# Moving two SBUF buffers of a fused attention and feed-forward kernel by 64 bytes, and what lies behind them by 256

## What is computed

```python
k_p = k.reshape(B, H, 72, 8, D).mean(axis=3)          # v_p likewise
attn = softmax(q @ k_p.T / sqrt(D)) @ v_p
h = x @ w_in;  g = maximum(0.01 * h, h);  y = g @ w_out          # layer 1
h = y @ w_in2; g = h * clip(h + 3, 0, 6) / 6;  out = g @ w_out2  # layer 2
```

## Time and profile before

| | us |
|---|---|
| median of three runs | 1704.76 |
| lowest, highest | 1704.0, 1704.78 |
| the profiled execution | 1704.56 |
| its span, first to last instruction | 1702.8 |
| TensorE matmuls busy | 1675.4 (98%) |
| VectorE busy | 1007.7 (59%) |
| ScalarE busy | 627.9 (37%) |
| GpSimd busy | 395.3 (23%) |

### The profile page before, as it was taken

How to read it: one execution, slowest core, us unless ns; L and a number is a source line. 1 busy time by engine, 2 the same in 40 slices (tenths; PEclk the granted TensorE clock), 3 DMA queues, 4 the chain that set the end, 5 groups by cost and what they waited for, 6 DMA issues and landing times. The chain is left out here.

```text
span 1702.8 us, 32933 instructions
## 1 busy us (share of the span) xinstructions
PE 1675.4 (98%) x10460; PEld 1489.4 (87%) x10460; DVE 1007.7 (59%) x1807; ACT 627.9 (37%) x1329; POOL 395.3 (23%) x427
## 2 busy tenths in 40 slices
PE   7999999999999999999999999999999999999999
PEld 6777888888888888888999888988989898989898
DVE  6767777676676867765455555444545454444444
ACT  4544433333333433333323333333333333333333
POOL 6226551021120212112432112121111212121200
PEclk8999999999999999999999999999999999999999
DMA  6745778768686786858787757666756675757562
GB/s 197 244 154 195 260 253 247 234 202 278 197 260 222 227 261 204 273 179 280 234 271 245 251 174 227 175 222 176 223 180 222 174 226 174 227 173 227 173 202 75
DMA packets 215810, 366.83 MB, mean 215 GB/s; under 512 B 22464, under 2 KB 47040, under 8 KB 215744
## 3 DMA queue, kind: packets, MB, share of 16 engines
q1 hardware_dynamic: 215744, 366.04, 68.1%
HBM read 308.28 MB, written 57.67 MB: 215 GB/s over the span
## 5 line engine op out<-in xcount | busy, mean ns | idle before, releaser
L1431 PE MATMUL ps_h<-xs_hi,ring 128*128 128x256 f32 x3808 | 814.8, 283 | 10.6 <-ACT p L1056 4.9
L1431 PEld LDWEIGHTS ps_h<-xs_hi,ring 128*128 128x128 f32 x3808 | 642.8, 189 | 56.4 <-issue 15.9
L1431 PE MATMUL ps_h<-xs_lo,ring 128*128 128x256 f32 x1904 | 534.3, 281 | 0.0
L1431 PEld LDWEIGHTS ps_h<-xs_lo,ring 128*128 128x128 f32 x1904 | 358.1, 188 | 25.7
L939 ACT ACTIVATE g_hi<-gate 128x512 fp32r<-128x512 f32 x288 | 181.9, 632 | 397.7 <-DVE gate L1137 212.7
L1384 PE MATMUL ps_y<-g_hi,wout_hi 128*128 128x512 f32 x576 | 225.7, 392 | 0.4 <-DVE y_stage L1192 0.4
L1386 PE MATMUL ps_y<-g_hi,wout_lo 128*128 128x512 f32 x576 | 225.4, 391 | 0.0
L1385 PE MATMUL ps_y<-g_lo,wout_hi 128*128 128x512 f32 x576 | 225.2, 391 | 0.0
L1196 DVE TENSOR_TENSOR u<-ps_h,p 128x256 f32<-128x256 f32 x272 | 114.3, 420 | 186.8 <-PE ps_h L1431 152.1
L1385 PE MATMUL ps_y<-wout_lo,g_hi 128*128 128x512 f32 x576 | 224.2, 389 | 0.0
L1386 PE MATMUL ps_y<-wout_hi,g_lo 128*128 128x512 f32 x576 | 224.2, 389 | 0.0
(11 more groups left out here) (115 smaller groups left out, 1994.2 us busy)
## 6 DMA issues: line engine op xcount, KB each, us to landing
ring<-w_in_split SPq DMA_DIRECT2D x920, 256.0 KB, 2.8
w_in_split<-ring SPq DMA_DIRECT2D x56, 256.0 KB, 3.5
w_in_split<-stage SPq DMA_DIRECT2D x56, 256.0 KB, 3.6
k_raw<-in_kT SPq DMA_DIRECT2D x32, 288.0 KB, 3.8
q_raw<-in_qT SPq DMA_DIRECT2D x32, 288.0 KB, 5.3
v_raw<-in_v SPq DMA_DIRECT2D x32, 288.0 KB
x0T<-x_stage SPq DMA_DIRECT2D x32, 288.0 KB, 3.8
x1T<-y_stage SPq DMA_DIRECT2D x36, 256.0 KB, 5.0
```

Source lines behind the costliest of these rows:

```text
L1431: mm = pe.matmul(banks[BANK_OF[r]], a, b[:, r, c, :], start=r in OPENS and c == 0 and n == 0, stop=c == 1 and n == 2, skip_group_check=True)
```

## The change

Sixteen float32 per partition (64 bytes) are allocated ahead of `g_hi`, and 48 (192 bytes) ahead of `x_stage`. Nothing reads or writes them. No instruction is added, removed or reordered.

```diff
         pre = sb("pre", [P, 2, N])
+
+        sb("pad_g", [P, 16])
         g_hi = sb("g_hi", [P, G_SLOTS, N], F32R)
         g_lo = sb("g_lo", [P, G_SLOTS, N], F32R)
+        sb("pad_x", [P, 48])
         x_stage = sb("x_stage", [P, DC, N])
```

## The result

The changed kernel takes 1712.61 us in the median of six runs (1712.09 to 1718.89), the kernel before 1704.77 us (six runs, 1704.0 to 1706.82). The ratio is 1.0049, with a 95% interval of 1.0038 to 1.006: slower by 0.5%, inside the forecast's range and against its likeliest case. The profiled execution has a span of 1711.5 us, 8.7 more than before, at a mean granted clock of 0.995 of full speed (0.996 before), so the clock is not what changed.

What follows compares the result with a forecast made beforehand. TensorE's matmuls, busy 98% of the span, were taken as the bound, so time is their number times the distance between starts. All terms were 0 against 1704.56 us; forecast 1704.7 us, likeliest case 1703 to 1707, whole range 1688 to 1720.

Steps and rivals of the forecast that it cites:

- likeliest case: Whole kernel: no effect on TensorE's pace, 1703 to 1707 us, chance 0.50.
- What writes g on ScalarE and VectorE: g_hi's copy and g_lo's operation at moved addresses: 0, bounds 20 ns an operation either way, hidden under TensorE's work.
- What of it is on the path: ScalarE's late p, once in a tile, 11 waits: 0.2 us either way, taken as 0.
- TensorE's reads: Matmuls of g with w_out, 64 bytes apart after the change: taken as 0, bounds +31 and -23 us.
- The 256 bytes: Buffers moved by 256 bytes keep their place modulo 256: taken as 0, upper bound a 4.9 us wait.
- The slower rival: g's matmuls always held up, 230 instead of 226 ns: +14 us, 1719 us, up to +31; chance 0.25.
- Its evidence for: For the slower pace: tile 0's xp, 64 bytes from the ring, takes 235 ns an interval.
- its evidence against: Against the slower pace: tile 0's g, at equal offsets with w_out, takes 235 ns as well.
- the first g group behind a steady run of xs: Place in TensorE's stream where the slower pace was to be decided: g's starts 230 instead of 226 ns apart.
- The faster rival: TensorE: g and xs at the same offset fast together, xs 114 instead of 118 ns, at most -23 us; chance 0.25.
- The exchange of paces: TensorE's earlier timeline: xs fast when g is slow and the other way round, 114 and 230 against 118 and 226 ns.
- The rule about the SBUF: Skill pages: TensorE never waits for another engine at SBUF, banks are partition groups; by it 0, given no chance from the rivals.

Runs made afterwards that it cites:

- g128_x256: Against the kernel before: g moved by 128 bytes, the buffers from x_stage on by 256; 1707.67 us, ratio 1.001.
- s64: Against the kernel before: xs and xp moved 64 bytes on, level with the ring, g left in place towards w_out; 1719.22 us, ratio 1.0075.
- ghi64: Against the kernel before: g_hi moved 64 bytes on, g_lo kept at its old place modulo 256; 1712.99 us, ratio 1.0054.
- s128: Against the kernel before: xs and xp moved 128 bytes on, g left in place towards w_out; 1712.88 us, ratio 1.0043.
- g0_x256: Against the kernel before: only the buffers from x_stage on moved, by 256 bytes, g left in place; 1705.47 us, ratio 0.9995.
- g192_x256: Against the kernel before: g moved 192 bytes on, the buffers from x_stage on and first-batch unit 3 by 256; 1708.41 us, ratio 1.002.
- g256_x256: Against the kernel before: g and all behind it moved by 256 bytes, first-batch unit 3 too; 1705.99 us, ratio 1.0003.
- all64: Against the kernel before: one pad ahead of everything, every buffer moved by 64 bytes, all relations kept; 1706.32 us, ratio 0.9998.
- w64_g64: Against the kernel before: g moved 64 bytes as in the change, w_out moved 64 with it; 1705.74 us, ratio 1.0003.

## Why the prediction was wrong, point by point

1. **What writes g on ScalarE and VectorE, taken as 0: right.** 632, 692 and 693 ns in the median, before and after.
2. **What of it is on the path, 0.2 us either way: right.** The stall for p became smaller, not by a faster g_hi but most likely because TensorE was slower: 3.4 us against 4.9.
3. **TensorE's reads, taken as 0: this is the step that failed.** It took from the earlier trace rows that xp with ring, 64 bytes apart, and g with w_out, at equal offsets, had 235 ns each in the same microsecond, and concluded "the slower pace there is the time's, not the offset's". The observation is right, the conclusion isn't. The runs show that a matmul's pace depends on its neighbours' operands as well as its own: g128_x256 makes untouched xs matmuls faster, s64 makes untouched g matmuls slower, and in ghi64 the g_lo that kept its place is as slow as g_hi. So does tile 0: with xp level with the ring (s64) xp falls from 233.5 to 228.8 ns and the g matmuls among it from 231.4 to 228.5. The slow pace was in good part xp's offset, passed on to a g that lay well. The geometry was not the later one either: 64 apart modulo 128 is 192 of 256 bytes for xp and 64 for the changed g, and by g128_x256 and s128 the relations do not repeat after 128. The term was worth 6.8 + 8.6 us on g and -3.1 us on xs.
4. **The 256 bytes, taken as 0: right.** g0_x256 is the kernel before.

**The slower rival** had the cause: g at 64 bytes from w_out held up in every matmul. Its evidence for, that xp is slow in rows 8, was sound by s64, and its evidence against, that g is equally slow there, was in good part the neighbour's effect. It priced it at 4 ns x 3456 = +14 us; the g matmuls do cost 4.5 ns more in the mean, +15.4 us. What it left out are two things given back, 3.1 us by faster xs matmuls and 3.3 us by shorter waits, so the median moved by 7.8 us and not by 14. It also named the place, the first g group behind a steady run of xs, and that is where the timeline shows it.

**The faster rival** expected g and xs, at the same distance from their weights, to be fast together. They aren't: with both level with their weights (s64) the kernel is 0.75% slower, with both 64 bytes off them, g above and xs below (the change itself), 0.5%, and with both 64 below (g192_x256) 0.2%. The exchange of paces it rested on is real: it is in g128_x256, xs 115.5 and g 232.2 ns, and does come from an address there. But in layer 2 the two effects cancel (a cycle of 1386.7 ns, as before), and in layer 1 they don't even do that (1394.5 against 1386.7), where 10 us less were expected.

The rule about the SBUF that stood beside the third point, the Trainium skill's page "SBUF — State Buffer", section "Door 1: The DMA port swizzle", divides the memory by partitions, so that by it a shift along the partition changes nothing for TensorE. The measurement differs: 64 bytes along the partition change g's matmuls in layer 2 from 226.8 to 231.8 ns. The measurement decides. That TensorE waits for another engine at the SBUF, which the section "Who interferes with whom" excludes, is not shown either: the relations found to count here are all between buffers that TensorE itself reads.

The chances rested on no row showing an address choose between the two paces. That was true of the rows: they hold one placement for each kind of matmul in its usual company, so they could not show it either way, and half the chance for no effect was more than they carried.

**What stays open.** Shown is that g's relation to w_out, modulo 256 bytes, is what costs the 8 us, and that the matmuls of a cycle change each other's pace. That the collision is between the moving stream and the loading of the next weights is an argument and not shown: these are the two kinds of TensorE work that the trace has, they overlap, and the matmul's duration by tile grew (389 to 397 ns in layer 1) while the weight load's stayed at 188. Why 256, and why xs does best at 192 from its ring while g and xp do best level with w_out and the ring, no run tells. The high and low parts of w_out and of xs were not moved one by one.

## What to carry to other kernels

Where TensorE has work back to back, a buffer inserted in SBUF is not free of charge even if no instruction changes: compare the distance from start to start of each kind of matmul before and after, as a mean over hundreds, since 4 ns in 227 are invisible in a single line. Write down the place of each moving and each stationary buffer relative to the others, insert in multiples of 256 bytes to stay neutral (here both shifts by 256 were, g0_x256 and g256_x256, and so was all64, which moves everything), or move partners together, as in w64_g64. And don't read one pair's pace from matmuls in other company.

## What the runs showed of the hardware that was not expected

- The same float32r matmul, in the same order and at full granted clock, starts 226.4 to 233.5 ns apart (512 columns, mean of layer 2) or 115.5 to 119.1 ns (256 columns), by the relations of the addresses modulo 256 bytes alone. The span of the kernel's time over these placements is 1704.8 to 1727.0 us, 1.3%.
- The effect couples neighbours: a cycle of nine matmuls has the same mean to 0.2 ns in the four kernels with the old relations (1386.7, 1386.8, 1386.9 and 1386.8 ns in layer 2), a moved g changes xs, and a moved xp changes the g matmuls among it (231.4 to 228.5 ns, s64).
- Xs matmuls have been seen at 113.3 ns in the mean (the last of the six in g128_x256's layer 2; the first has 120), and g matmuls at 226.8 in the mean, in the kernel before. Together, as an estimate from these two, they would make a cycle of 6 x 113.3 + 3 x 226.8 = 1360 ns, 2% less than 1386.7. No placement tried has both, and none beats the kernel before; g128_x256 only comes level with it in layer 2.
